# Gated scan and ELU feed-forward in fp32: another turn of PSUM banks in the first block, and one gate moved on VectorE

## What is computed

```python
sig = 1.0 / (1.0 + np.exp(-f_logit))
f = lower_bound + (1.0 - lower_bound) * sig
for t in range(S):                      # per batch and channel
    h = f[:, t] * h + (1 - f[:, t]) * x[:, t]
    y[:, t] = h
...
h = y @ w_in                            # 256 -> 2048
g = np.where(h > 0.0, h, np.exp(np.minimum(h, 0.0)) - 1.0)
out = g @ w_out                         # 2048 -> 256
```

## Time and profile before

| | us |
|---|---|
| runs | 992.01, 992.06, 992.34 |
| median | 992.06 |
| profiled execution, its time | 991.67 |
| profiled execution, span of the records | 989.8 |
| TensorE busy | 983.3 |
| ScalarE busy | 791.4 |
| VectorE busy | 727.9 |
| GpSimd busy | 631.7 |

### The profile page before, as it was taken

One profiled execution on the slowest core, in us unless ns is written; L12 is line 12 of the kernel. 1 busy time (PEld: TensorE's weight loads), 2 busy tenths in 40 slices (PEclk: granted clock), 3 DMA queues, 4 the chain that ended last, 5 costly groups with the idle time before them and its releaser, 6 DMA issues.

```text
span 989.8 us, 15352 instructions
## 1 busy us (share of the span) xinstructions
PE 983.3 (99%) x4362; PEld 816.4 (82%) x4362; DVE 727.9 (74%) x915; ACT 791.4 (80%) x1425; POOL 631.7 (64%) x474
## 2 busy tenths in 40 slices
PE   8999999999999999999999999999999999999998
PEld 6887888888888888888888888888888888888997
DVE  6995876886786697688679668758867957875544
ACT  7987878877887887888787787787888788778775
POOL 2586887567657557656755855765775575576454
PEclk9999999999999999999999999999999999999999
DMA  7202002101201100210210120011021012000001
GB/s 276 66 24 72 33 1 75 54 1 53 74 0 40 55 32 0 74 53 0 63 64 0 42 64 21 19 56 52 0 68 59 0 46 70 0 0 13 33 1 38
DMA packets 23211, 41.88 MB, mean 42 GB/s; under 512 B 2704, under 2 KB 4240, under 8 KB 23184
## 3 DMA queue, kind: packets, MB, share of 16 engines
q1 hardware_dynamic: 22752, 41.04, 12.8%
q10 hardware_dynamic: 432, 0.53, 0.2%
HBM read 29.10 MB, written 12.45 MB: 42 GB/s over the span
## 4 chain that ended last, share of the span: by engine, by line
PE 99%; DMA 1%; DVE 0%; issue 0%; ACTq 0%; ACT 0%
PE acc L864 17%; PE acc L862 17%; PE acc L863 17%; PE h L834 14%; PE h L836 14%; PE h L838 14%; PE h L957 1%; PE h L959 1%; PE h L958 1%; DMA x<-value 1%; PE h L938 0%; DVE x L603 0%; PE h L929 0%; PE acc L959 0%; PE acc L957 0%; PE acc L938 0%
## 5 line engine op out<-in xcount | busy, mean ns | idle before, releaser
L317 POOL TENSOR_TENSOR g_lo<-e,g_hi 128x512 fp32r<-128x512 f32 (+1 forms) x384 | 519.3, 1361 | 352.4 <-ACT g_hi L458 351.0
L444 ACT ACTIVATE e<-h 128x512 f32<-128x512 f32 (+1 forms) x380 | 226.0, 595 | 149.5 <-PE h L838 117.0
L694 DVE SCALAR_TENSOR_TENSOR e<-e,h 128x512 f32<-128x512 f32 (+1 forms) x380 | 256.8, 676 | 76.8 <-ACT e L450 76.4
L864 PE MATMUL acc<-g_hi,w_out_lo 128*128 128x512 f32 (+1 forms) x768 | 297.3, 387 | 0.0
L862 PE MATMUL acc<-g_hi,w_out_hi 128*128 128x512 f32 (+1 forms) x768 | 297.3, 387 | 0.0
L863 PE MATMUL acc<-g_lo,w_out_hi 128*128 128x512 f32 (+1 forms) x768 | 297.2, 387 | 0.0
L458 ACT CAST g_hi<-e 128x512 fp32r<-128x512 f32 (+1 forms) x384 | 232.6, 606 | 22.7 <-DVE e L694 22.7
L450 ACT ACTIVATE e<-e 128x512 f32<-128x512 f32 (+1 forms) x384 | 241.5, 629 | 8.4
L834 PE MATMUL h<-a_hi,w_in_hi 128*128 128x512 f32 (+1 forms) x616 | 238.8, 388 | 0.0
L836 PE MATMUL h<-a_lo,w_in_hi 128*128 128x512 f32 (+1 forms) x616 | 238.4, 387 | 0.0
L838 PE MATMUL h<-a_hi,w_in_lo 128*128 128x512 f32 (+1 forms) x616 | 238.3, 387 | 0.0
(11 more groups left out here) (72 smaller groups left out, 568.0 us busy)
## 6 DMA issues: line engine op xcount, KB each, us to landing
out<-out_sb SPq DMA_DIRECT2D x44, 256.0 KB, 2.0
gate<-forget_logit SPq DMA_DIRECT2D x43, 256.0 KB, 2.6
x<-value SPq DMA_DIRECT2D x43, 256.0 KB, 2.7
w_in_raw<-w_in SPq DMA_DIRECT2D x8, 256.0 KB, 6.1
w_out_raw<-w_out SPq DMA_DIRECT2D x8, 256.0 KB, 7.1
x<-value SPq DMA_DIRECT2D x4, 224.0 KB, 2.5
gate<-forget_logit SPq DMA_DIRECT2D x4, 224.0 KB, 2.5
out<-out_sb SPq DMA_DIRECT2D x4, 224.0 KB, 1.9
```

Of the source, the lines that this page charges most:

```text
L317: nc.gpsimd.tensor_tensor(g_lo[:, t % RING, 0:w], e[:, t % TILES, 0:w], g_hi[:, t % RING, 0:w].bitcast(F32), ALU.subtract).then_inc(g_lo_r ...
L444: nc.scalar.activation(e[:, i, 0:w], bank_of(j, t)[:, 0:w], ACT.Relu, scale=-1.0).then_inc(r_ready, 1)
L694: nc.vector.scalar_tensor_tensor(e[:, t % TILES, 0:w], e[:, t % TILES, 0:w], -1.0, bank_of(j, t)[:, 0:w], ALU.add, ALU.max).then_inc(g_rea ...
L864: done = nc.tensor.matmul(bank, lo, g_hi[:, t % RING, 0:w], start=False, stop=closes)
```

## The change

Two edits. In the first block, tiles 14 to 27 take the banks of `h` in another cyclic order: by t % 4 from tile 14 on, 1, 0, 3, 2 instead of 3, 0, 1, 2. Tiles 28 to 31 keep 3, 2, 3, 1. Since the wait of a product is derived from the list, the tile that it waits for changes with it. In the steady blocks, the instruction `open_gate(n, 1, 0)` (the first half of batch 1 of the next block) leaves place (2, 2) of VectorE's list, where it stood behind `weigh(n, 0, 1)` and ahead of `add_c22`, and goes to a new place (2, 3), behind the ELU of C12 and ahead of the ELU of C22 in group q = 2. The call for place 3 is made in every group and does something only in q = 2.

```diff
-FIRST_BANK = ([1, 2, 3, 0, 4, 5, 1, 2, 3, 0, 1, 2, 4, 5] + [(3, 0, 1, 2)[t % TILES] for t in range(UNITS - 2)]
+FIRST_BANK = ([1, 2, 3, 0, 4, 5, 1, 2, 3, 0, 1, 2, 4, 5] + [(1, 0, 3, 2)[t % TILES] for t in range(UNITS - 2)]
               + [3, 2, 3, 1])
...
                 if at == (2, 2):
                     weigh(n, 0, 1)
+                if at == (2, 3):
                     open_gate(n, 1, 0)
...
                     elu(j, t + C12)
+                    spare(j, par, q, 3, last)
                     elu(j, t + C22)
```

## The result

The changed kernel takes 990.51 us (median of 22 runs, 989.88 to 992.52) against 992.02 for the kernel before, measured beside it. The ratio is 0.9985 (95% interval 0.9979 to 0.9991), so it is 0.15% faster. One of the 22 executions of the kernel before took 2749.38, which the median does not feel. The forecast was 990.47, with a range of 990.0 to 991.3. The profiled execution took 990.41.

The account below looks back on a forecast made before the run. TensorE, busy 99% of the span, was taken to bound the kernel. Removing 0.87 us in the first block and 0.72 in the steady blocks, 1.59 in all, takes 992.06 to 990.47, range 990.0 to 991.3.

Parts of the forecast that it names:

- The two losses: TensorE waits to be removed: 0.87 us at tile 28, and nine times 0.08, or 0.72, at P4 in q = 2.
- listed signs of being wrong: Gap ahead of tile 14 or 30, late P2 or P3 in q = 3, 1.5 us gate delaying C22's ELU, span falling too little.
- Tile 28: First block: it would wait for tile 24 instead of 26, with 3.4 us left, so the 0.87 us go.
- Tile 14: First block: it would wait for tile 10 instead of 8, released 0.77 us ahead of its matmul; cost 0.
- The spare part: At tile 14: of the margin about 0.19 us is needed, leaving 0.58 us to spare.
- Tile 30: First block: still waits for tile 28 in bank 3, with 0.65 us left even if that ELU did not move; cost 0.
- The gate's new place: VectorE, q = 2, behind the ELU of C12: gate takes 0.60 us, hidden in the wait for ScalarE; cost 0, upper bound 1.51.
- The rival of q = 3: Another release, nearest P3 in q = 3, takes over the steady blocks' 0.08, the weigh meeting GpSimd's subtraction: 991.19, chance 0.05.
- The 0.91: Extra time of a gate beside GpSimd's work, taken as the weigh's price in q = 3; add_u4 would keep 0.29 us.
- The chance for "slower": Whole kernel slower by over 0.2%: 0.02; faster by over 0.2% was 0.08, within 0.90.
- The slower rival: Tile 14's new predecessor late by D costs D - 0.58 us, outweighing the gain from D = 2.17; chance 0.02, half visibly slower.

Follow-up runs that it names:

- run 2: Only the gate moved, banks of tiles 14 to 27 as before, against the kernel before: 991.29 us, ratio 0.9992.
- run 1: Only the new turn of banks, gate left ahead of add_c22, against the kernel before: 991.18 us, ratio 0.999.
- Run 3: Against the kernel before: gate moved, tiles 14 to 27 in the old bank order, only tile 28 sent to bank 1 instead of 3: 990.44 us, ratio 0.9982.
- run 5: Changed kernel plus one fill of an unused tile on VectorE ahead of the ELU of tile 10: 990.61 us.
- run 6: Changed kernel plus one scan of an unused 128 x 512 tile ahead of the ELU of tile 10: 992.08 us.
- Run 4: Changed kernel with the gate back ahead of add_c22 in q = 2 and the weigh moved between the two ELUs instead: 990.48 us, ratio 0.9985.
- run 7: Changed kernel plus one 128 x 512 scan behind the moved gate, ahead of the ELU of C22, in ten blocks: 990.78 us.
- run 8: Changed kernel plus two scans behind the moved gate, ahead of the ELU of C22, in ten blocks: 1005.75 us.
- run 9: Changed kernel with the 1 KB load of the lower bound issued by GpSimd instead of on ScalarE's queue: 992.07 us, ratio 1.0003 to the kernel before.

## Why the prediction was right

- **The two losses.** Both were read from start times and both were right in place and size: 0.87 at tile 28 (it stays in run 2 and goes in runs 1 and 3), and 0.72 in the ten blocks (816.73 us in run 1, 816.00 in run 2). One of the listed signs of being wrong did appear, a span that falls by less than the two gaps; it came from the later start of the stream, not from a gap.
- **Tile 28.** The wait for tile 24 left 3.46 us (ELU ends 73.78, matmul 77.24). Run 3 shows that only this predecessor mattered.
- **Tile 14.** The margin was 0.78 in this execution, as in the trace of before (0.77). The spare part worked out as 0.58 is bracketed by runs 5 and 6: a margin of 0.40 costs nothing, and a release that is late costs its lateness and 0.21.
- **Tile 30.** Forecast to keep at least 0.65. It kept 0.90: due at 82.68, the ELU of 28 ended at 81.78.
- **The gate's new place.** Forecast 0.60 in VectorE's wait for ScalarE, measured 0.54. Run 4 shows that the old place was slow from the sum of two instructions held by GpSimd.
- **The rival of q = 3.** The collision of the weigh with GpSimd did come, but cost 0.20 (0.88 against 0.68 of that weigh before), not the 0.91 of its bound. P3's margin rose to 1.00. The 0.91 was no upper bound: the weigh of q = 2 took 1.79, which is 1.11 more than 0.68, and 1.11 in q = 3 would have left P3 about 0.09, less than it needs. It was luck in the timing that the subtraction was nearly over when the weigh of q = 3 began. The weigh ended at 206.19, 0.55 after GpSimd's subtraction, and the scan ahead of it ended at 204.21, 1.08 after the subtraction beside it (203.13). The Trainium skill, SBUF — State Buffer, "Who interferes with whom", says that a VectorE instruction with two SBUF inputs and a GpSimd instruction that reads SBUF shut each other out, and the later one waits for the whole of the earlier. The traces agree: the scan took 2.33 here and 1.68 in run 7, and ended 1.08 behind the subtraction in both (204.70 against 203.62 in run 7). And P3 is not the next to be late: run 8 shows P2, by way of the fork on ScalarE. The prediction named P2 only among what would show it wrong; the price that it gave a late release held, the wait that it called the nearest did not.
- **The rest.** The forecast median was 990.47 and the measured one 990.51. That they agree to 0.04 is partly luck: runs 3 and 4, with no gap either, gave 990.44 and 990.48, but the two parts alone came out 0.06 and 0.10 larger than forecast. The chance for "slower" was given as 0.02, where the rivals listed add up to 0.01 (half of the 0.02 for tile 14). The slower rival needed tile 14's ELU late by 2.17 us to undo the gain: run 6, with an ELU late by 2.13 (38.45 was its time against the stream), came to 992.08.

## What to carry to other kernels

When one engine is busy 99% of the span, read the start times of its instructions, not their durations or the idle column: waits shorter than the overlap of two records leave no idle time in the row of the matmuls. The wait of the weight load names their place, and the count of instructions times the time from start to start gives their size (here to 0.01 us). Price a moved instruction by what runs beside it at the old and at the new place; the same gate took 1.51 beside GpSimd and 0.54 in its pause. For a wait on a tile further back, work out the new predecessor of every tile, since one entry may carry the whole gain, and add a known delay on the chip to learn which release is next.

## What the runs showed of the hardware

**The margin of a wait.** A release 0.35 to 0.44 us ahead of the matmul cost nothing (0.35 at P3 and 0.44 at tile 10 before, 0.40 in run 5); one 0.11 ahead cost 0.08; one 0.67 late (tile 28 before) cost 0.87, and one 1.35 late cost 1.56. So in each of these the release was needed about 0.2 us early. After the two real stops about half of that lies between the release and the matmul (40.58 to 40.67 in run 6), and the rest in the matmuls behind it, of which the first two come 0.31 and 0.24 behind one another instead of 0.227.

**TensorE's clock.** In the traced execution of run 9 TensorE did nothing from 8 to 10 us, having run its warm-up matmuls (on a zeroed tile, ahead of the first product) until then. The windows view (busy time of each engine, then the granted clock) shows what followed:

```profile
8.00:10.00 2.00, 0.00 (x0) 0.00 (x0) 1.96 (x3) 1.75 (x4) 0.00 (x0) 1.00 1.05 405
10.00:12.00 2.00, 1.89 (x5) 1.51 (x6) 1.97 (x3) 1.76 (x5) 0.00 (x0) 0.51 1.06 409
12.00:13.00 1.00, 1.00 (x4) 0.81 (x3) 1.00 (x2) 0.49 (x1) 0.00 (x0) 0.50 1.04 399
14.00:16.00 2.00, 2.00 (x10) 1.63 (x10) 0.90 (x2) 0.37 (x1) 0.00 (x0) 1.00 1.05 405
```

From 10 to 13 us the granted clock was 0.51 and 0.50, the 1.2 GHz level, and 1.00 from 14 us on. In the traced execution of the changed kernel TensorE was idle for 1.52 us at the same point, and it stayed at 1.00:

```profile
8.24 1.24 PE L931 MATMUL h<-a_hi,w_in_hi 128*128 128x512 f32 x4 [1.52 <-ACT a_hi L419]
```

The idle time is not the only difference between the two: from 4 to 6 us TensorE ran 6 warm-up matmuls in run 9 and 11 in the changed kernel. So that the longer pause brought the clock down is likely, but not shown. Nor does it happen each time: the mean granted clock was 0.998 in five of the eleven executions of run 9, and in one of the 22 of the changed kernel (992.52 us). In those five the 1 KB load cost twice, once as a delay and once in the clock of the first products.

**A small load by GpSimd.** Issued at 1.31, it was in use at 6.17, 4.86 us later. By ScalarE's queue it was issued at 0.75 and in use at 3.88, 3.13 later. The large loads ran beside both, so the runs don't say how much of the 1.7 us is GpSimd's own way of issuing.
